# Second phase: z transposed by VectorE and DRAM, the down product three tiles behind

## The chip, the cores and the metric

The kernel runs on one core of a Trainium2 chip. The metric is the device time in microseconds of one execution. Before the change it is 914.69 us, the median of three runs (914.66 to 915.95).

## The reference

Retention (batch 4, 8 heads, 768 positions, head size 64) is followed by two dense blocks over the 3072 tokens, each with 512 features in and out.

```
state = gamma * state + k_t v_t^T ;  y_t = scale * q_t state        # attention
h = x @ w_in (512 x 2048) ; g = h clamped to [-1, 1] and blended with a square ; x = g @ w_out
h = x @ w_in (512 x 1024)
e = exp(h - max(h)) ; solu = h * e / (sum(e) + 1e-9)
z = (solu - mean) / sqrt(var + 1e-6)
out = (z * g_ln) @ w_out (1024 x 512)
```

Only the second dense block (the last four lines) is touched by the change.

## The kernel before

All products are done in f32 split into a high and a low part (`split`, `passes`): a product is three matmuls, hi x hi, hi x lo and lo x hi, so the splits of every operand are made by ScalarE (the high part, a copy that rounds) and by VectorE or POOL (the low part, a subtraction).

The first phase (`first_phase`) does attention and the first dense block for six blocks of 512 tokens and stores its result x2, transposed, in DRAM. In its last block it also loads and splits the weights of the second dense block.

The second phase (`second_phase`) goes over 24 tiles of 128 tokens. For each tile:
- TensorE `up(t, n)`: h for 128 tokens x 1024, in two halves of 512 columns, 12 matmuls each, into one of two PSUM tensors `h2_0`, `h2_1`. It waits for `h2_used` of tile t-2, that is for solu of that tile.
- VectorE and ScalarE in turn: `h_max` (L787), `neg_max` (L789), exp on ScalarE (L752), the sum and its inverse (L792, L795), `solu` (L797), `neg_mean` (L800), square on ScalarE (L755), `var` (L805), the power -0.5 on POOL (L818), and `z` (L808).
- TensorE `flip(t)` (L694): eight transposes of 128x128, that is matmuls of z with an identity, into the PSUM tensor `zT_ps`.
- `split_z(t)`: ScalarE copies the two halves of `zT_ps` as `zT_hi` (L727, through the helper `copy`) and VectorE subtracts for `zT_lo` (L776).
- TensorE `down(t)` (L706): 24 matmuls of zT with w_out into `o_ps`; ScalarE copies the result to `o` and SP stores it (L655).

Each engine works through a queue written out by hand. TensorE does up(t, 0), flip(t-1), up(t, 1), down(t-1). VectorE and ScalarE begin tile t with `split_x`, in ten of the tiles (the split of the next pair of x2 tiles, L770 on VectorE), then with split_z(t-1), and go on to tile t. SP loads x2 for two tiles (L650) when the products of an earlier pair have ended, and stores the outputs. In tile 0 the last two down products of the first phase and its evacuations are put in (`finish`).

There is one `z`, one `zT`, and two slots of `o` and `x2`. The SBUF of the second phase lies over weights of the first (`place`).

Of the kernel before, what the change touches and what calls it, by code (L numbers as in the profile page):

```python
# [5 lines left out]
F32 = mybir.dt.float32  # L6
# [54 lines left out]
def place(nc):  # L61
# [26 lines left out]

    plain("ident", [P, P])
    plain("g_ln", [P, FT2])  # L90
# [42 lines left out]
    plain("o", [P, 2, DM])  # L133
    split("zT", [P, FT2, P])
    assert cursor[0] <= w_at + 9 * 8192
    return mem


def first_phase(nc, block, io, sem, mem, x2_dram, finish):
    w, w_raw, x, y, g, gate = (mem[n] for n in ("w", "w_raw", "x", "y", "g", "g_raw"))  # L140
    tables, state, half_bias, ident = (mem[n] for n in ("tables", "state", "half_bias", "ident"))
    kn_scale = tables[:, 0:H]
# [6 lines left out]
    with ExitStack() as ctx:  # L149
# [419 lines left out]
        def _(pool):  # L569
# [28 lines left out]
            def dense(blk):  # L598
                for f in range(FT1):
# [8 lines left out]
                    if blk == BLOCKS - 1 and 12 <= f < FT1:  # L608
                        for piece in (2 * (f - 12), 2 * (f - 12) + 1):
# [4 lines left out]

            nc.gpsimd.memset(ident[:, :], 0.0).then_inc(sem["ident"], 1)
            pool.wait_ge(sem["ident"], 1)
            nc.gpsimd.affine_select(out=ident[:, :], in_=ident[:, :], compare_op=ALU.not_equal, fill=1.0, base=0,
                                    pattern=[[-1, P]], channel_multiplier=1).then_inc(sem["ident"], 1)
            for f in range(W_READY):
# [7 lines left out]

def second_phase(nc, block, io, sem, mem, x2_dram, finish):
# [3 lines left out]
    w_in, w_out, g_ln = mem["w2_in"], mem["w2_out"], mem["g_ln"]  # L632
    x_raw, x = [mem["x2_0_raw"], mem["x2_1_raw"]], [mem["x2_0"], mem["x2_1"]]
    e, solu, dev, z, zT, o, power, ident = (
        mem[n] for n in ("e", "solu", "dev", "z", "zT", "o", "power", "ident"))
    with ExitStack() as ctx:
        hp = [ctx.enter_context(nc.psum_tensor(f"h2_{i}", [P, FF2], F32)) for i in range(2)]
        tp = ctx.enter_context(nc.psum_tensor("zT_ps", [P, FF2], F32))
        op = [ctx.enter_context(nc.psum_tensor(f"o_ps{i}", [P, DM], F32)) for i in range(2)]
# [4 lines left out]
        @block.sync  # L644
        def _(sp):
            def load_x2(n):
                wait(sp, sem["h2_ready"], 4 * n - 4)
                for m in range(KT):
                    wait(sp, sem["x2_stored"][m], 16 * (n // 2 + 1))
                sp.dma_start(x_raw[n % 2][:, :, :], x2_view[:, :, n * 2 * P:(n + 1) * 2 * P])\  # L650
                    .then_inc(sem["x2_loaded"][n % 2], 16)

            def store(t):
                sp.wait_ge(sem["o_ready"], t + 1)
                sp.dma_start(io["out"][t], o[:, t % 2, :]).then_inc(sem["o_stored"][t % 2], 16)  # L655

            for pair in range(TILES // 2):
                if pair + 2 < TILES // 2:
                    load_x2(pair + 2)
                store(2 * pair)  # L660
                store(2 * pair + 1)
            for par in range(2):
                sp.wait_ge(sem["o_stored"][par], 16 * (TILES // 2))

        @block.tensor
        def _(pe):
            mm = nc.tensor.matmul

            def up(t, n):
                if n == 0:  # L670
                    if t == 0:
                        pe.wait_ge(sem["probs"], 2 * CHUNKS)
                        pe.wait_ge(sem["y_done"], LATER)
                        pe.wait_ge(sem["state_added"], UPDATES)
                        pe.wait_ge(sem["w2_in_lo"], KT)
                    if t == 1:
                        pe.wait_ge(sem["gmax"], BLOCKS * FT1)
                    wait(pe, sem["h2_used"], t - 1)
                    wait(pe, sem["x2_lo"], t // 2 + 1)
                cols = slice((t % 2) * P, (t % 2 + 1) * P)  # L680
                for kt in range(KT):
                    for i, (xx, ww) in enumerate(passes(x[t // 2 % 2], w_in)):
                        last = mm(hp[t % 2][:, SEGS[n]], xx[:, kt, cols], ww[:, kt, SEGS[n]],  # L683
                                  start=kt == 0 and i == 0, stop=kt == KT - 1 and i == 2)
                last.then_inc(sem["h2_ready"], 1)

            def flip(t):
# [3 lines left out]
                pe.wait_ge(sem["z_ready"], t + 1)  # L691
                wait(pe, sem["zT_lo"], 2 * t)
                for f in range(FT2):
                    last = nc.tensor.transpose(tp[:, f * P:(f + 1) * P], z[:, f * P:(f + 1) * P], ident[:, :])  # L694
                    if f % 4 == 3:
                        last.then_inc(sem["zT_ready"], 1)

            def down(t):
# [24 lines left out]

        @block.scalar
        def _(act):
# [19 lines left out]
            for t in range(TILES):  # L745
                if t >= 2 and t % 2 == 0 and t // 2 + 1 < TILES // 2:
                    split_x(t // 2 + 1)
                if t:
                    split_z(t - 1)
                act.wait_ge(sem["neg_max"], t + 1)  # L750
# [6 lines left out]
                if t == 0:  # L757
                    finish["act_evacuate"]()
                else:
                    output(t - 1)  # L760
            split_z(TILES - 1)
            output(TILES - 1)

        @block.vector
        def _(dve):
# [7 lines left out]
            def split_z(t):  # L773
                for n in range(2):
                    dve.wait_ge(sem["zT_hi"], 2 * t + n + 1)
                    tt(zT[1][:, 4 * n:4 * n + 4, :], tp[:, SEGS[n]].rearrange("p (f t) -> p f t", f=4),  # L776
                       zT[0][:, 4 * n:4 * n + 4, :].bitcast(F32), ALU.subtract).then_inc(sem["zT_lo"], 1)

            dve.wait_ge(sem["power_set"], 1)
            for t in range(TILES):  # L780
                if t >= 2 and t % 2 == 0 and t // 2 + 1 < TILES // 2:
                    split_x(t // 2 + 1)
                if t:
                    split_z(t - 1)
                h = hp[t % 2][:, :]
# [16 lines left out]
                if t == 0:  # L802
# [19 lines left out]
SEMAPHORES = {  # L822
    1: ("first_mask mask_loaded tables gains ident half_set power_set state_zeroed x0_hi x0_lo "
        "kn_scaled s_ready probs y_ready y_done ku_ready state_added state_decayed w_hi w_in_lo w_out_lo "
        "x_hi x_lo h_ready clamped squared gmax g_hi g_lo g_used "
        "w2_in_hi w2_in_lo w2_scaled w2_out_hi w2_out_lo x2_hi x2_lo h2_ready h2_used z_ready zT_ready zT_hi "
        "zT_lo o_done o_ready h_max neg_max e_ready e_sum_eps e_inv neg_mean sq_sum var rstd"),
    2: "acc_free x2_loaded o_stored",
    4: "x2_stored w2_in_loaded",
# [6 lines left out]
def build(nc, io):  # L836
    x2_dram = nc.dram_tensor("x2T", (DM, TOKENS), F32).ap()
    with ExitStack() as ctx:
        sem = {}
# [57 lines left out]
```

## Time and profile before

| | us |
|---|---|
| median of three runs | 914.69 |
| profiled execution, its own time | 917.66 |
| its span, first to last instruction | 915.9 |
| TensorE busy (PE) | 898.3 |
| VectorE busy (DVE) | 386.5 |
| ScalarE busy (ACT) | 281.9 |
| POOL busy | 211.9 |

The mean granted clock of TensorE is 0.996 of full speed. The second phase begins at about 617 us. In the profile, PE is TensorE, PEld its weight loads, DVE is VectorE, ACT is ScalarE, POOL is GpSimd and SPq the queue of SyncE, which issues the DMAs. The durations of successive matmuls overlap, so the distance between their starts tells how long one holds the engine.

### The profile page before, as it was taken

The numbers are of one execution on the slowest core, as the hardware profiler recorded it, in microseconds if no ns is written. First come the engines' busy times: TensorE is split into PE (matmuls) and PEld (weight loads), VectorE is DVE, ScalarE is ACT, GpSimd is POOL, SyncE is SP. The second block draws the span as 40 slices with busy tenths as digits, with TensorE's granted clock in tenths as the row PEclk, the third lists the DMA queues.
The fourth block names the chain that finished last, engine by engine and source line by source line (L and its number), as shares of the span: only waits on it lengthen the run. The fifth ranks groups of instructions, "written<-read, shape, count | busy, mean of one in ns | idle before, by whom it ended". The sixth has DMA issues, their size and how long they took to land.

```text
span 915.9 us, 12101 instructions
## 1 busy us (share of the span) xinstructions
PE 898.3 (98%) x5056; PEld 742.2 (81%) x5056; DVE 386.5 (42%) x642; ACT 281.9 (31%) x438; POOL 211.9 (23%) x187
## 2 busy tenths in 40 slices
PE   6999999999999999999999999999999999999997
PEld 5788888888888888888888888887888888888885
DVE  4544443334333343334322343535554455445542
ACT  2433332213212232122212243343333333333332
POOL 2554532322222322322212122252000000000000
PEclk9999999999999999999999999999999999999998
DMA  9812111111121111110111032202111111111100
GB/s 346 320 59 70 47 47 47 48 57 35 58 69 59 47 47 47 56 49 24 58 58 35 1 108 93 76 1 70 47 47 47 43 37 37 47 47 47 47 24 23
DMA packets 33462, 57.68 MB, mean 63 GB/s; under 512 B 3328, under 2 KB 9472, under 8 KB 33408
## 3 DMA queue, kind: packets, MB, share of 16 engines
q1 hardware_dynamic: 33120, 56.38, 17.9%
q8 instruction: 40, 0.66, 0.3%
q10 hardware_dynamic: 288, 0.53, 0.2%
q14 instruction: 14, 0.11, 0.0%
HBM read 44.31 MB, written 12.58 MB: 62 GB/s over the span
## 4 chain that ended last, share of the span: by engine, by line
PE 95%; issue 2%; DVE 1%; ACT 1%; POOL 1%; DMA 1%; POOLq 0%; SPq 0%; ACTq 0%
PE acc L338 30%; PE h L325 28%; PE h L683 14%; PE o_ps L706 13%; PE att L266 3%; PE att L279 2%; PE zT_ps L694 2%; PE att L282 2%; PE att L295 1%; DMA q<-in_q 1%; POOL w L595 0%; PE acc L279 0%; PE h L266 0%; ACT w L365 0%; POOL kn L576 0%
## 5 line engine op out<-in xcount | busy, mean ns | idle before, releaser
L338 PE MATMUL acc<-g_hi,w 128*128 128x512 f32 x768 | 256.7, 395 | 0.0
L325 PE MATMUL h<-x_hi,w 128*128 128x512 f32 x768 | 252.4, 390 | 3.9 <-DVE x_lo L454 2.1
L604 POOL TENSOR_TENSOR g_lo<-g_raw,g_hi 128x512 fp32r<-128x512 f32 x96 | 123.2, 1284 | 404.9 <-ACT g_hi L365 404.9
L414 ACT ACTIVATE g_raw<-g_raw,half_bias 128x512 f32<-128x512 f32 x96 | 69.5, 724 | 348.0 <-DVE g_raw L539 348.0
L325 PEld LDWEIGHTS h<-x_hi,w 128*128 128x128 f32 x768 | 144.2, 188 | 34.4 <-ACT x_hi L365 2.4
L338 PEld LDWEIGHTS acc<-g_hi,w 128*128 128x128 f32 x768 | 144.1, 188 | 33.2 <-issue 0.7
L338 PE MATMUL acc<-g_lo,w 128*128 128x512 f32 x384 | 149.8, 390 | 0.0
L325 PE MATMUL h<-x_lo,w 128*128 128x512 f32 x384 | 149.4, 389 | 0.0
L539 DVE TENSOR_SCALAR g_raw<-h 128x512 f32<-128x512 f32 x96 | 66.4, 691 | 185.1 <-PE acc L338 184.4
L544 DVE TENSOR_TENSOR g_raw<-h,g_raw 128x512 f32<-128x512 f32 x96 | 66.4, 692 | 62.3 <-ACT g_raw L414 61.7
L325 PEld LDWEIGHTS h<-x_lo,w 128*128 128x128 f32 x384 | 72.1, 188 | 14.9
L338 PEld LDWEIGHTS acc<-g_lo,w 128*128 128x128 f32 x384 | 72.1, 188 | 13.9
L365 ACT ACTIVATE g_hi<-g_raw 128x512 fp32r<-128x512 f32 x96 | 60.7, 632 | 72.8 <-DVE g_raw L544 72.8
L706 PE MATMUL o_ps<-w_out_hi,zT_hi 128*128 128x512 f32 x192 | 75.8, 395 | 1.7 <-DVE zT_lo L776 1.7
L683 PE MATMUL h<-w_in_hi,x_hi 128*128 128x512 f32 x192 | 76.6, 399 | 0.0
L706 PE MATMUL o_ps<-w_out_hi,zT_lo 128*128 128x512 f32 x192 | 75.4, 393 | 0.0
L706 PE MATMUL o_ps<-w_out_lo,zT_hi 128*128 128x512 f32 x192 | 75.4, 393 | 0.0
L683 PE MATMUL h<-w_in_hi,x_lo 128*128 128x512 f32 x192 | 75.0, 391 | 0.0
L683 PE MATMUL h<-w_in_lo,x_hi 128*128 128x512 f32 x192 | 74.8, 390 | 0.0
L818 POOL TENSOR_TENSOR rstd<-var,power 128x1 f32<-128x1 f32 x24 | 13.1, 548 | 263.3 <-DVE var L805 263.3
L752 ACT ACTIVATE e<-h,neg_max 128x1024 f32<-128x1024 f32 x24 | 26.8, 1117 | 84.0 <-DVE neg_max L789 84.0
L776 DVE TENSOR_TENSOR zT_lo<-zT_ps,zT_hi 128x512 fp32r<-128x512 f32 x48 | 31.0, 687 | 32.3 <-ACT zT_hi L727 32.2
(72 smaller groups left out, 899.4 us busy)
## 6 DMA issues: line engine op xcount, KB each, us to landing
kT<-in_kT SPq DMA_DIRECT2D x24, 256.0 KB, 2.7
q<-in_q SPq DMA_DIRECT2D x24, 256.0 KB, 2.7
v<-in_v SPq DMA_DIRECT2D x24, 256.0 KB, 2.9
x2T<-y SPq DMA_DIRECT2D x24, 256.0 KB, 2.5
x_raw<-x2T SPq DMA_DIRECT2D x12, 512.0 KB, 3.7
out<-o SPq DMA_DIRECT2D x24, 256.0 KB, 2.0
kn<-in_kn SPq DMA_DIRECT2D x20, 256.0 KB, 3.6
w_raw<-in_moe_w_in SPq DMA_DIRECT2D x16, 256.0 KB, 9.5
```

Of the source, the lines that this page charges most:

```text
L266: last = mm(out[e][:, p * P:(p + 1) * P], kT[half(e), p, :], q[half(e), p, :], start=True, stop=True)
L325: last = mm(hb[f % 2][:, :], ww, xx[:, kt, :], start=kt == 0 and t == 0, stop=kt == KT - 1 and t == 2)
L338: last = mm(acc[m][:, :], ww, gg[:, f % 2, :], start=f == 0 and t == 0, stop=f == FT1 - 1 and t == 2)
L365: return nc.scalar.activation(out, in_, ACT.Copy)
L414: nc.scalar.activation(gate[:, f % 2, :], gate[:, f % 2, :], ACT.Square, bias=half_bias[:, 0:1], scale=0.5).then_inc(sem["squared"], 1)
L539: nc.vector.tensor_scalar(gate[:, f % 2, :], h, 1.0, -1.0, ALU.min, ALU.max)\
L544: tt(gate[:, f % 2, :], h, gate[:, f % 2, :], ALU.max).then_inc(sem["gmax"], 1)
L604: tt(g[1][:, f % 2, :], gate[:, f % 2, :], g[0][:, f % 2, :].bitcast(F32), ALU.subtract)\
L683: last = mm(hp[t % 2][:, SEGS[n]], xx[:, kt, cols], ww[:, kt, SEGS[n]], start=kt == 0 and i == 0, stop=kt == KT - 1 and i == 2)
L706: last = mm(op[t % 2][:, :], zz[:, f, :], ww[:, f, :], start=f == 0 and i == 0, stop=f == FT2 - 1 and i == 2)
L752: nc.scalar.activation(e[:, :], hp[t % 2][:, :], ACT.Exp, bias=st("neg_max", t), accum_out=st("e_sum", t)).then_inc(sem["e_ready"], 1)
L776: tt(zT[1][:, 4 * n:4 * n + 4, :], tp[:, SEGS[n]].rearrange("p (f t) -> p f t", f=4), zT[0][:, 4 * n:4 * n + 4, :].bitcast(F32), ALU.subtr ...
```

## The change

TensorE no longer transposes. VectorE transposes z in squares of 32x32, right behind z, into `zq` (`zq[i*32+r, q, f, c]`, where i is the group of 32 tokens and q the group of 32 features within 128). SP stores `zq` (512 KB) to DRAM, waits until it has landed, and loads it in four DMAs of 128 KB, one for each group of 32 partitions, in runs of 1 KB, as `zt`, in which the 32-token groups stand side by side. ScalarE and VectorE split `zt`, now from SBUF, into one of three `zT`. `zq` and `zt` have two slots.

The down product of tile t-3 (`LAG2`) now follows the whole up product of tile t. VectorE does split_z(t-1) at the end of tile t, behind the transpose of z(t); ScalarE does it at the end of tile t too, behind square(t) and the output of tile t-3. On SP the turn of tile t stands behind the store of output t-3. The identity and its two POOL instructions go. Without `zT_ps`, `o_ps0` and `o_ps1` come to lie two PSUM banks earlier.

```diff
+LAG2 = 3
+SQ = 32
@@ place
-    split("zT", [P, FT2, P])
-    assert cursor[0] <= w_at + 9 * 8192
+    plain("zq", [P, 2, P // SQ, FT2, SQ])
+    plain("zt", [P, 2, P // SQ, FT2, SQ])
+    for n in range(LAG2):
+        split(f"zT{n}", [P, FT2, P])
+    assert cursor[0] <= w_at + 13 * 8192
@@ first_phase, POOL
-            nc.gpsimd.memset(ident[:, :], 0.0).then_inc(sem["ident"], 1)
-            pool.wait_ge(sem["ident"], 1)
-            nc.gpsimd.affine_select(out=ident[:, :], ...)
@@ second_phase, SP
-            for pair in range(TILES // 2):
-                if pair + 2 < TILES // 2:
-                    load_x2(pair + 2)
-                store(2 * pair)
-                store(2 * pair + 1)
+            def turn(t):
+                sp.wait_ge(sem["zq_ready"], t + 1)
+                wait(sp, sem["zt_loaded"][t % 2], 64 * (t // 2))
+                sp.dma_start(z_dram[t % 2], zq[:, t % 2, :, :, :].rearrange("p q f c -> p (q f c)"))\
+                    .then_inc(sem["zq_stored"][t % 2], 16)
+                sp.wait_ge(sem["zq_stored"][t % 2], 16 * (t // 2 + 1))
+                wait(sp, sem["zT_lo"], 2 * t - 2)
+                squares = z_dram[t % 2].rearrange("(i r) (q x) -> q r i x", r=SQ, q=P // SQ)
+                for q in range(P // SQ):
+                    sp.dma_start(zt[q * SQ:(q + 1) * SQ, t % 2, :, :, :].rearrange("r i f c -> r i (f c)"),
+                                 squares[q]).then_inc(sem["zt_loaded"][t % 2], 16)
+
+            for t in range(TILES):
+                if t % 2 and t // 2 + 2 < TILES // 2:
+                    load_x2(t // 2 + 2)
+                if t >= LAG2:
+                    store(t - LAG2)
+                turn(t)
+            for t in range(TILES - LAG2, TILES):
+                store(t)
@@ second_phase, TensorE
-                up(t, 0)
-                if t >= 2:
-                    flip(t - 1)
-                up(t, 1)
+                up(t)
                 if t == 0:
                     finish["down"]()
-                if t == 1:
-                    flip(0)
-                if t:
-                    down(t - 1)
-            flip(TILES - 1)
-            down(TILES - 1)
+                if t >= LAG2:
+                    down(t - LAG2)
+            for t in range(TILES - LAG2, TILES):
+                down(t)
@@ second_phase, ScalarE
             def split_z(t):
-                wait(act, sem["o_done"], t)
+                act.wait_ge(sem["zt_loaded"][t % 2], 64 * (t // 2 + 1))
+                wait(act, sem["o_done"], t - LAG2 + 1)
                 for n in range(2):
-                    act.wait_ge(sem["zT_ready"], 2 * t + n + 1)
-                    copy(zT[0][:, 4 * n:4 * n + 4, :], tp[:, SEGS[n]].rearrange("p (f t) -> p f t", f=4))\
-                        .then_inc(sem["zT_hi"], 1)
+                    fs = slice(4 * n, 4 * n + 4)
+                    copy(zT[t % LAG2][0][:, fs, :].rearrange("p f (i c) -> p f i c", c=SQ),
+                         zt[:, t % 2, :, fs, :].rearrange("p i f c -> p f i c")).then_inc(sem["zT_hi"], 1)
...
-                if t:
-                    split_z(t - 1)
                 act.wait_ge(sem["neg_max"], t + 1)
...
-                else:
-                    output(t - 1)
+                if t >= LAG2:
+                    output(t - LAG2)
+                if t:
+                    split_z(t - 1)
+            output(TILES - 3)
             split_z(TILES - 1)
+            output(TILES - 2)
             output(TILES - 1)
@@ second_phase, VectorE
-                if t:
-                    split_z(t - 1)
                 h = hp[t % 2][:, :]
...
+                dve.wait_ge(sem["z_ready"], t + 1)
+                wait(dve, sem["zq_stored"][t % 2], 16 * (t // 2))
+                nc.vector.transpose(zq[:, t % 2, :, :, :].rearrange("p q f c -> p f q c"),
+                                    z[:, :].rearrange("p (f q c) -> p f q c", q=P // SQ, c=SQ))\
+                    .then_inc(sem["zq_ready"], 1)
+                if t:
+                    split_z(t - 1)
             split_z(TILES - 1)
```

## Rows read from the trace of the kernel before

**Rows 1.** The page: busy time by engine, and the chain's shares.
```profile
PE 898.3 (98%) x5056; PEld 742.2 (81%) x5056; DVE 386.5 (42%) x642; ACT 281.9 (31%) x438; POOL 211.9 (23%) x187
...
PE 95%; issue 2%; DVE 1%; ACT 1%; POOL 1%; DMA 1%; POOLq 0%; SPq 0%; ACTq 0%
```

**Rows 2.** Timeline, a steady tile on TensorE: start us, us, engine, line, operation.
```profile
785.03 1.03 PE L694 MATMUL zT_ps<-ident,z 128*128 128x128 f32 x8
...
788.64 0.39 PE L706 MATMUL o_ps<-w_out_hi,zT_hi 128*128 128x512 f32 x1
...
794.08 0.39 PE L683 MATMUL h<-w_in_hi,x_hi 128*128 128x512 f32 x1
...
796.82 1.04 PE L694 MATMUL zT_ps<-ident,z 128*128 128x128 f32 x8
```

**Rows 3.** Timeline, tiles 0 and 1.
```profile
622.48 0.39 PE L338 MATMUL acc<-g_hi,w 128*128 128x512 f32 x1
...
631.81 0.81 DVE L808 TENSOR_SCALAR z<-solu,neg_mean,rstd 128x1024 f32<-128x1024 f32 x1 [0.74 <-POOL rstd L818]
...
633.13 0.39 PE L683 MATMUL h<-w_in_hi,x_lo 128*128 128x512 f32 x1
...
635.37 0.50 PE L706 MATMUL o_ps<-w_out_hi,zT_hi 128*128 128x512 f32 x1 [0.98 <-DVE zT_lo L776]
```

**Rows 4.** Timeline, the end on TensorE.
```profile
899.88 0.39 PE L706 MATMUL o_ps<-w_out_hi,zT_lo 128*128 128x512 f32 x1
...
905.08 0.77 PE L706 MATMUL o_ps<-w_out_hi,zT_hi 128*128 128x512 f32 x1 [0.71 <-DVE zT_lo L776]
...
909.06 0.48 PE L706 MATMUL o_ps<-w_out_hi,zT_hi 128*128 128x512 f32 x1
...
912.36 0.39 PE L706 MATMUL o_ps<-w_out_hi,zT_lo 128*128 128x512 f32 x1
```

**Rows 5.** Busy time by stretch, the end (PEclk: granted clock).
```profile
901.00:916.00 15.00, 9.64 (x32) 7.46 (x32) 2.19 (x3) 1.96 (x4) 0.50 (x1) 0.77 0.09 35
```

**Rows 6.** Timeline, a steady tile on VectorE.
```profile
786.36 1.29 DVE L776 TENSOR_TENSOR zT_lo<-zT_ps,zT_hi 128x512 fp32r<-128x512 f32 x2 [0.68 <-ACT zT_hi L727]
...
788.84 1.22 DVE L787 TENSOR_REDUCE h_max<-h 128x1 f32<-128x1024 f32 x1 [1.20 <-PE h L683]
...
791.91 1.28 DVE L797 SCALAR_TENSOR_TENSOR solu<-e,e_inv,h 128x1024 f32<-128x1024 f32 x1
...
795.52 0.81 DVE L808 TENSOR_SCALAR z<-solu,neg_mean,rstd 128x1024 f32<-128x1024 f32 x1 [0.66 <-POOL rstd L818]
```

**Rows 7.** Groups by line of VectorE and POOL: busy us, mean ns.
```profile
L770 DVE TENSOR_TENSOR x_lo<-x_raw,x_hi 128x1024 fp32r<-128x1024 f32 x10 | 12.2, 1219 | 0.0
...
L524 DVE TENSOR_TENSOR x_lo<-x_raw,x_hi 128x1024 fp32r<-128x1024 f32 x1 | 1.5, 1472 | 1.6 <-ACT x_hi L365 1.6
...
L604 POOL TENSOR_TENSOR g_lo<-g_raw,g_hi 128x512 fp32r<-128x512 f32 x96 | 123.2, 1284 | 404.9 <-ACT g_hi L365 404.9
```

**Rows 8.** DMAs: median us to landing by line, four issues in row, the x2 load.
```profile
out<-o SPq DMA_DIRECT2D x24, 256.0 KB, 2.0
...
x2T<-y SPq DMA_DIRECT2D x4, 256.0 KB, 3.1
...
631.40 1.88 SPq L202 DMA_DIRECT2D x2T<-y  x4
...
L650 SPq DMA_DIRECT2D x_raw<-x2T x10: 371/377/378, 633.6 to 847.7; - x10
...
DMA to landing us min/median/max: 3.5/3.6/4.9
```

**Rows 9.** ScalarE: the output copy in a tile, groups of copies.
```profile
794.58 0.57 ACT L727 ACTIVATE o<-o_ps 128x512 f32<-128x512 f32 x1
...
L365 ACT ACTIVATE g_hi<-g_raw 128x512 fp32r<-128x512 f32 x96 | 60.7, 632 | 72.8 <-DVE g_raw L544 72.8
...
L727 ACT ACTIVATE zT_hi<-zT_ps 128x512 fp32r<-128x512 f32 x48 | 26.2, 595 | 47.0 <-PE zT_ps L694 47.0
```

More of the change, by code:

```diff
@@ L87, in split_in_place @@
         mem[f"{name}_raw"] = put(f"{name}_raw", shape, F32, at=at)
-    plain("ident", [P, P])
     plain("g_ln", [P, FT2])
@@ L140, in first_phase @@
     w, w_raw, x, y, g, gate = (mem[n] for n in ("w", "w_raw", "x", "y", "g", "g_raw"))
-    tables, state, half_bias, ident = (mem[n] for n in ("tables", "state", "half_bias", "ident"))
+    tables, state, half_bias = (mem[n] for n in ("tables", "state", "half_bias"))
     kn_scale = tables[:, 0:H]
@@ L625, in _, with second_phase @@
                 dense(blk)
-def second_phase(nc, block, io, sem, mem, x2_dram, finish):
+def second_phase(nc, block, io, sem, mem, x2_dram, z_dram, finish):
     TILES = TOKENS // P
@@ L631, in second_phase @@
     x2_view = x2_dram.rearrange("(kt p) t -> p kt t", p=P)
-    w_in, w_out, g_ln = mem["w2_in"], mem["w2_out"], mem["g_ln"]
+    w_in, w_out = mem["w2_in"], mem["w2_out"]
     x_raw, x = [mem["x2_0_raw"], mem["x2_1_raw"]], [mem["x2_0"], mem["x2_1"]]
-    e, solu, dev, z, zT, o, power, ident = (
-        mem[n] for n in ("e", "solu", "dev", "z", "zT", "o", "power", "ident"))
+    e, solu, dev, z, zq, o, power = (mem[n] for n in ("e", "solu", "dev", "z", "zq", "o", "power"))
+    zT, zt = [mem[f"zT{n}"] for n in range(LAG2)], mem["zt"]
     with ExitStack() as ctx:
         hp = [ctx.enter_context(nc.psum_tensor(f"h2_{i}", [P, FF2], F32)) for i in range(2)]
-        tp = ctx.enter_context(nc.psum_tensor("zT_ps", [P, FF2], F32))
         op = [ctx.enter_context(nc.psum_tensor(f"o_ps{i}", [P, DM], F32)) for i in range(2)]
@@ L667, in _, with up, down @@
             mm = nc.tensor.matmul
[L669 to L675, printed above, removed]
-                    if t == 1:
-                        pe.wait_ge(sem["gmax"], BLOCKS * FT1)
-                    wait(pe, sem["h2_used"], t - 1)
-                    wait(pe, sem["x2_lo"], t // 2 + 1)
-                cols = slice((t % 2) * P, (t % 2 + 1) * P)
[L681 to L687, printed above, removed]
+            def up(t):
+                if t == 0:
+                    pe.wait_ge(sem["probs"], 2 * CHUNKS)
+                    pe.wait_ge(sem["y_done"], LATER)
+                    pe.wait_ge(sem["state_added"], UPDATES)
+                    pe.wait_ge(sem["w2_in_lo"], KT)
+                if t == 1:
+                    pe.wait_ge(sem["gmax"], BLOCKS * FT1)
+                wait(pe, sem["h2_used"], t - 1)
+                wait(pe, sem["x2_lo"], t // 2 + 1)
+                cols = slice((t % 2) * P, (t % 2 + 1) * P)
+                for seg in SEGS:
+                    for kt in range(KT):
+                        for i, (xx, ww) in enumerate(passes(x[t // 2 % 2], w_in)):
+                            last = mm(hp[t % 2][:, seg], xx[:, kt, cols], ww[:, kt, seg],
+                                      start=kt == 0 and i == 0, stop=kt == KT - 1 and i == 2)
+                last.then_inc(sem["h2_ready"], 2)
+            def down(t):
                 if t == 0:
@@ L690, in flip @@
                         pe.wait_ge(sem["acc_free"][par], 2 * BLOCKS)
[L691 to L698, printed above, removed]
                 wait(pe, sem["o_ready"], t - 1)
@@ L704, in down @@
                         pe.wait_ge(sem["w2_out_lo"], f + 1)
-                    for i, (zz, ww) in enumerate(passes(zT, w_out)):
+                    for i, (zz, ww) in enumerate(passes(zT[t % LAG2], w_out)):
                         last = mm(op[t % 2][:, :], zz[:, f, :], ww[:, f, :],
@@ L774, in split_z @@
                 for n in range(2):
+                    fs = slice(4 * n, 4 * n + 4)
                     dve.wait_ge(sem["zT_hi"], 2 * t + n + 1)
-                    tt(zT[1][:, 4 * n:4 * n + 4, :], tp[:, SEGS[n]].rearrange("p (f t) -> p f t", f=4),
-                       zT[0][:, 4 * n:4 * n + 4, :].bitcast(F32), ALU.subtract).then_inc(sem["zT_lo"], 1)
+                    hi, lo = (part[:, fs, :].rearrange("p f (i c) -> p f i c", c=SQ) for part in zT[t % LAG2])
+                    tt(lo, zt[:, t % 2, :, fs, :].rearrange("p i f c -> p f i c"), hi.bitcast(F32), ALU.subtract)\
+                        .then_inc(sem["zT_lo"], 1)
             dve.wait_ge(sem["power_set"], 1)
@@ L822 @@
 SEMAPHORES = {
[L823 removed]
+    1: ("first_mask mask_loaded tables gains half_set power_set state_zeroed x0_hi x0_lo "
         "kn_scaled s_ready probs y_ready y_done ku_ready state_added state_decayed w_hi w_in_lo w_out_lo "
         "x_hi x_lo h_ready clamped squared gmax g_hi g_lo g_used "
[L826 removed]
+        "w2_in_hi w2_in_lo w2_scaled w2_out_hi w2_out_lo x2_hi x2_lo h2_ready h2_used z_ready zq_ready zT_hi "
         "zT_lo o_done o_ready h_max neg_max e_ready e_sum_eps e_inv neg_mean sq_sum var rstd"),
[L828 removed]
+    2: "acc_free x2_loaded o_stored zq_stored zt_loaded",
     4: "x2_stored w2_in_loaded",
@@ L837, in build @@
     x2_dram = nc.dram_tensor("x2T", (DM, TOKENS), F32).ap()
+    z_dram = [nc.dram_tensor(f"z{n}", (P, FF2), F32).ap() for n in range(2)]
     with ExitStack() as ctx:
@@ L847, in build @@
         first_phase(nc, block, io, sem, mem, x2_dram, finish)
-        second_phase(nc, block, io, sem, mem, x2_dram, finish)
+        second_phase(nc, block, io, sem, mem, x2_dram, z_dram, finish)
 def kernel(q, k, v, moe_w_in, moe_w_out, moe2_w_in, moe2_w_out, moe2_g_ln):
```

3 lines of the change are left out of this document (removed).

## The prediction

> **What bounds the kernel now.** I read the page's busy shares and chain first, then the second phase closely, since nothing before 617 us changes but two small POOL instructions. TensorE is busy 98% of the span and is 95% of the chain that ended last [rows 1]: its instructions set the time, and other engines matter only where it waits. In a steady tile TensorE never stops: 24 products take 794.08 - 788.64 = 5.44 us (0.2267 each), so a tile's 48 cost 10.88; a tile is 796.82 - 785.03 = 11.79 long; the other 0.91 is the eight transposes [rows 2]. So they are paid in full on the bounding engine, though they overlap among themselves (eight in 1.03).
>
> **The sum for TensorE.** What is not product in the second phase:
> - Start: up(1) ends at 633.13 + 0.23 = 633.36, the first down product starts at 635.37: 2.0 us of flip(0) and of the wait for zT_lo [rows 3].
> - Steady: from 635.37 + 5.44 = 640.81 to 899.88 + 0.23 = 900.11 lie 22 flips and 22 x 10.88 = 239.4 us of products; the other 19.9 is 0.90 a tile [rows 3, 4].
> - End: from 900.11 to 905.08 TensorE waits for z(23), flips and waits for zT_lo: 5.0 us. The last 24 products then take 912.59 - 905.08 = 7.51 instead of 5.44: their first nine start 0.43 apart (the granted clock of this stretch is 0.77, so part of it ran at 1.2 GHz), 2.1 us [rows 4, 5].
>
> Together 29.0 us. Check: from 622.48 (up(0) done) 48 half tiles of 5.44 are 261.1, ending at 883.6; plus 29.0 is 912.6, where the trace has it. With TensorE never waiting the span would be 883.6 + 3.3 (912.59 to the end of the span: output copy and store [rows 4]) = 886.9, or 29.0 less: the most that the change can give.
>
> **What the change puts in place of it: VectorE.** One new VectorE pass (T) a tile, a round trip through DRAM (R), and the split copies now read SBUF. T isn't in the trace. VectorE passes over 128x1024 f32 take 1.22 (the reduce of h_max), 1.22 (x_lo) and, the scaling that makes z, 0.81; 1.47 is the slowest; far off, POOL needs 1.28 for 512, that is 2.57 for 1024 [rows 6, 7]. So the bounds are 0.8 and 2.6; I take T = 1.25, a little above the two at 1.22, which it is nearest to: one tensor read and one written, in blocks.
>
> VectorE's queue in a tile, counted from D(t), the start of h_max(t):
> - z ends at D + 7.49 (788.84 to 795.52 + 0.81) [rows 6]; the passes between wait for ScalarE's exp and square and for POOL's power, and don't change.
> - + 0.04 + T transpose, - 0.08 (an independent successor starts that much early: two halves of 0.69 show as 1.29 [rows 6]) + 1.29 split_z(t-1), - 0.08: D(t+1) = D(t) + 8.66 + T = 9.91.
> - before ten of the tiles also split_x, 1.22 - 0.08 = 1.14 [rows 7]: 11.05.
>
> The mean is 10.43, against 10.88 of TensorE: VectorE is 96% filled and nearly the bound, where it had over 1 us a tile free. It also starts late: the new order gives TensorE up(1), up(2), up(3) back to back (633.36, 638.80, 644.24), while z(0) ends at 632.62 [rows 3], h_max(1) starts at 633.8, h_max(2) at 633.8 + 9.91 + 1.14 = 644.9, 6 us behind its product, h_max(3) at 654.8, 10.6 behind. Does TensorE feel it? up(4) starts at 644.24 + 5.44 = 649.7 and needs solu(2), done 4.4 us after h_max starts (791.91 + 1.28 against 788.84 [rows 6]), at 649.3: just in time. Then the lag shrinks, since VectorE is faster than TensorE. down(t-3), due when up(t) ends, needs split_z(t-3), which is done before h_max(t-1): enough. So I take no stall from tile 1 to 22.
>
> **The round trip R**, from the transpose's end to the last of four loads landed, behind one another on SP. The store is 512 KB: stores of 256 KB land 2.0 to 3.1 us after issue, the 512 KB load 3.6 (4.9 at most); I take 3.3. The four loads are issued about 0.45 apart (four x2T stores take 1.88) and the last (128 KB) lands 2.0 to 3.1 after its issue; I take 1.35 + 2.3. With 0.15 of SP between: R = 7.1; the ends are 2.0 + 1.35 + 2.0 + 0.1 = 5.5 and 4.9 + 1.4 + 4.9 + 0.1 = 11.3 [rows 8].
> R is hidden in the middle. ScalarE comes to split_z(t-1) at D(t) + 6.3, after square and output (794.58 + 0.57 in a tile with D = 788.84) [rows 9], that is 9.91 + 6.3 - 8.78 = 7.4 us after the transpose of t-1 ended; VectorE wants the first half at D(t) + 8.7, so ScalarE may start 1.8 later still. So R up to 9.2 costs nothing before the last tile. On SP the x2 load goes out behind the four loads, and the store of an output and the turn of the next tile behind it: it may land up to 1 us after ScalarE wants it, in ten tiles; with VectorE's lag that would cost up to 0.5 each, and I count 0.5 in all. The copies out of SBUF cost 0.63 instead of 0.60 [rows 9], beside other waits: nothing. POOL's two identity instructions at the start go: at most POOL's 1% of the chain, nearly all of it in later work, so nothing [rows 1]. Nobody else waits for the swap of PSUM banks.
>
> **The end.** D(23) = 633.8 + 22 x 9.91 + 10 x 1.14 = 863.3, + 0.5 = 863.8; up(23) ends at 644.24 + 20 x 10.88 = 861.8. z(23) at 871.3, transposed 872.6, landed 879.7, first half copied and split 881.1 (0.60 + 0.69 + 0.1). TensorE has down(20), (21), (22) until 861.8 + 3 x 5.44 = 878.2, so it waits 2.9 us before down(23), which ends at 886.5; + 3.3 = 889.8. That is 26.1 below the span of 915.9. After the wait of 2.1 us and the transposes the clock had fallen in the run before; a wait of 2.9 may do the same, 0 to 2.1 us, and I take 1. So -25.1. The profiled execution took 917.66 us (its span and 1.76 around it), 2.97 above the median of the runs shown; I carry the difference to the median: 914.69 - 25.1 = 889.6.
>
> **The rivals.**
> 1. *The transpose pass is dear* (T well over 1.3). VectorE's queue is the pace, so each us of T above 1.25 costs 22 steps and the last tile, 23 to 24 us in all, one for one. T = 1.8 gives 889.6 + 13 = 903; T = 2.5 gives 918, slower than before; the break is at T = 2.3. For it: no row shows the operation, and the POOL row shows that a pass can need twice the time for an element. Against it: every VectorE pass over 1024 elements lies at or below 1.47 [rows 7]. The Trainium skill ("VectorE: DVE Perf Modes", The three transpose paths) gives 311 ns for 128 columns in bf16; times eight, an estimate by that page, is 2.49 us, and the kernel would be no faster. The Trainium skill elsewhere ("Vector Engine (DVE) Microarchitecture Reference", 3.8 The reshape front-end and per-opcode configuration) has the transpose at one element per cycle and lane, by which most of the 311 ns are fixed and T is an estimated 1.2 to 1.3; the trace of before decides neither.
> 2. *The round trip sets the pace* (R over 9.2), the one that can turn the sign by itself. ScalarE's queue then stops at split_z(t-1), and VectorE's behind it: D(t+1) = D(t-1) + 8.78 + R + 0.1 + 1.8, and 1.14 more in every other tile, so (R + 11.8)/2 a tile. R = 10 gives 10.9, 22 x 0.5 + 2.9 at the end + 2 at the start = 16 us, 905; R = 11 gives 11.4 and 25 + 3: 918, slower; it decides from R = 10.9. For it: the 4.9 us seen for a 512 KB load, and x2 loads and output stores on the same queue. Against it: 3.6 is the median of that load, and 2.0 that of the stores [rows 8]. The Trainium skill ("VectorE: DVE Perf Modes", The three transpose paths) warns that a plain DMA that transposes by strides is 19 times slower than the crossbar; here the rows moved are 1 KB whole, as in the x2 load that lands in 3.6 us [rows 8], so I don't apply it; if it held, it would be this rival.
> 3. *TensorE keeps most of its tile*: the pitch of 0.2267 is not kept where the transposes went, or VectorE's lag costs stalls in every tile (11.3 instead of 10.88): 22 x 0.4 = 9 us given back, 899. Against it: the 24 products beside VectorE and ScalarE work keep the pitch exactly [rows 2].
>
> **How the numbers follow.** The forecast 0.66; rival 1 0.14 (half of it under 903, 0.04 past the break); rival 2 0.13 (0.06 past the break); rival 3 0.07. The least is 914.69 - 29 = 885.7 (no wait at the end); the forecast's own range is 886 to 895 (T to 1.4, R to 8.5, clock 0 to 2). To hold 8 in 10 it reaches into rivals 1 and 3: 886 to 903. A difference under 0.2% (1.8 us) can't be told from none here. Faster by more: 0.66 + 0.07 + 0.09 + 0.06 = 0.88; within: 0.02; slower: 0.10.
>
> **What would show it.** Right: no L694 and a TensorE tile of 10.88 from tile 4 on; the VectorE transpose at 1.2 to 1.3 us; h_max 6 to 11 us behind its product at tiles 2 to 6 and under 3 at tile 23; four loads landed 6.5 to 8.5 us after the transpose; one wait of 2 to 4 us before the last down product and 9 or fewer slow products behind it. Wrong: waits of TensorE for solu or zT_lo in every tile (rival 1 if VectorE has no idle time before h_max, rival 2 if ScalarE waits for the loads), or a pitch over 0.23.

## The result, and the profile after

The changed kernel takes 890.2 us (median of four runs, 890.07 to 890.45) against 915.32 for the kernel before on the same chip: a ratio of 0.9713, with a 95% interval of 0.970 to 0.9727. The forecast was 889.6. Executions of the changed kernel differ by about 1.2 us with the mean granted clock, 1.00 or 0.998, so a difference under 1 us between two kernels here is none. The profiled execution has a span of 888.7 us, 27.2 under the 915.9 of the trace before.

The page of the changed kernel, busy time and chain, which answer to [rows 1]:

```profile
PE 873.4 (98%) x4864; PEld 719.5 (81%) x4864; DVE 411.9 (46%) x666; ACT 283.0 (32%) x438; POOL 211.6 (24%) x185
...
PE 67%; DVE 18%; issue 5%; ACT 4%; DMA 3%; POOL 2%; SPq 1%; POOLq 0%; ACTq 0%; DVEq 0%
```

TensorE is as full as before and has 192 instructions less. But the chain is now on VectorE, ScalarE and POOL for 24% of the span, most of the second phase: it is the chain through VectorE's queue, which just keeps up.

The timeline of TensorE: the start of up(2), the turns between down and up at the start, the start of down(20), and the rows with a wait:

```profile
632.72 0.39 PE L700 MATMUL h<-w_in_hi,x_hi 128*128 128x512 f32 x1
...
643.60 0.39 PE L715 MATMUL o_ps<-w_out_hi,zT_hi 128*128 128x512 f32 x1
...
649.52 0.50 PE L700 MATMUL h<-w_in_hi,x_hi 128*128 128x512 f32 x1 [0.32 <-DVE solu L804]
...
655.12 0.39 PE L715 MATMUL o_ps<-w_out_hi,zT_hi 128*128 128x512 f32 x1
660.56 0.39 PE L700 MATMUL h<-w_in_hi,x_hi 128*128 128x512 f32 x1
666.00 0.39 PE L715 MATMUL o_ps<-w_out_hi,zT_hi 128*128 128x512 f32 x1
...
861.84 0.39 PE L715 MATMUL o_ps<-w_out_hi,zT_hi 128*128 128x512 f32 x1
...
879.78 0.47 PE L715 MATMUL o_ps<-w_out_hi,zT_hi 128*128 128x512 f32 x1 [1.47 <-DVE zT_lo L785]
...
885.12 0.39 PE L715 MATMUL o_ps<-w_out_hi,zT_lo 128*128 128x512 f32 x1
```

A tile is 666.00 - 655.12 = 10.88 us, where it was 11.79 [rows 2]; from 655.12 to 861.84 there are 19 of them in 206.72 us, 10.88 each, and no wait. What is left that is not product: up(4) should start at 643.60 + 5.44 = 649.04 and down(1) follow at 654.48; it follows at 655.12, so 0.64 there. down(20) starts at 861.84, so the last of the 24 down products should start at 861.84 + 3 x 5.44 = 878.16 and starts at 879.78: 1.62. It takes 5.57 instead of 5.44. Together 2.4 us, where the kernel before had 29.0. That is 26.6 of the 27.2; the other 0.6 is the first phase, which ends at 616.4 instead of 617.0 (TensorE's first wait for a DMA and its waits for a weight were shorter), and isn't the change's: a second trace of the kernel before has 616.6.

VectorE, three tiles at the start and the last:

```profile
632.01 1.25 DVE L819 STREAM_TRANSPOSE zq<-z 128x1024 f32<-128x1024 f32 x1
...
645.11 1.22 DVE L794 TENSOR_REDUCE h_max<-h 128x1 f32<-128x1024 f32 x1
...
654.97 1.22 DVE L794 TENSOR_REDUCE h_max<-h 128x1 f32<-128x1024 f32 x1
...
862.37 1.22 DVE L794 TENSOR_REDUCE h_max<-h 128x1 f32<-128x1024 f32 x1
...
869.89 1.25 DVE L819 STREAM_TRANSPOSE zq<-z 128x1024 f32<-128x1024 f32 x1
871.06 1.25 DVE L785 TENSOR_TENSOR zT_lo<-zt,zT_hi 128x512 fp32r<-128x512 f32 x2
878.94 1.29 DVE L785 TENSOR_TENSOR zT_lo<-zt,zT_hi 128x512 fp32r<-128x512 f32 x2 [6.63 <-ACT zT_hi L731]
```

h_max(2) starts 6.9 us after its product ended (638.16), h_max(3) 11.4 after (643.60), h_max(23) 0.5 after (861.84). The lag builds up in the first three tiles and is worked off by the last. Before the change h_max waited 26.3 us in all for its products; now it never waits for one: but for 0.9 us at split_x(2), VectorE goes from tile to tile at its own pace, in 9.86 us, or 11.00 where split_x comes first.

SP and ScalarE around the last round trip:

```profile
871.17 0.34 SPq L662 DMA_DIRECT2D z<-zq  x1
873.80 1.75 SPq L668 DMA_DIRECT2D zt<-z  x4
```

```profile
878.28 1.15 ACT L731 ACTIVATE zT_hi<-zt 128x512 fp32r<-128x512 f32 x2 [4.77 <-DMA zt<-z]
```

The transpose ends at 871.14, ScalarE goes on at 878.28: R = 7.1.

### The profile page after: what moved, and what is told of

Its sections match the earlier page's. It is cut to its first block, busy times and chain, and to the rows that moved or that the text cites. A ratio compares the mean times of both kernels' runs of the same rounds, so it can differ in the third digit from the quotient of the medians.

```text
span 888.7 us, 11899 instructions
## 1 busy us (share of the span) xinstructions
PE 873.4 (98%) x4864; PEld 719.5 (81%) x4864; DVE 411.9 (46%) x666; ACT 283.0 (32%) x438; POOL 211.6 (24%) x185
## 2 busy tenths in 40 slices
DMA packets 50742, 82.84 MB, mean 93 GB/s; under 512 B 5248, under 2 KB 23680, under 8 KB 50688
## 4 chain that ended last, share of the span: by engine, by line
PE 67%; DVE 18%; issue 5%; ACT 4%; DMA 3%; POOL 2%; SPq 1%; POOLq 0%; ACTq 0%; DVEq 0%
PE acc L342 30%; PE h L329 29%; DVE solu L804 3%; DVE zq L819 3%; ACT e L755 3%; DVE h_max L794 3%; DVE zT_lo L785 3%; PE att L270 2%; PE att L283 2%; DVE z L815 2%; PE att L286 2%; POOL rstd L832 1%; DVE x_lo L777 1%; DMA mask<-in_mask 1%; PE att L299 1%
## 5 line engine op out<-in xcount | busy, mean ns | idle before, releaser
L700 PE MATMUL h<-w_in_hi,x_hi 128*128 128x512 f32 x192 | 74.8, 390 | 0.3 <-DVE solu L804 0.3
L715 PEld LDWEIGHTS o_ps<-w_out_hi,zT_hi 128*128 128x128 f32 x192 | 36.0, 188 | 9.4 <-issue 1.9
```

What stands on the lines that cost most here:

```text
L700: last = mm(hp[t % 2][:, seg], xx[:, kt, cols], ww[:, kt, seg], start=kt == 0 and i == 0, stop=kt == KT - 1 and i == 2)
L715: last = mm(op[t % 2][:, :], zz[:, f, :], ww[:, f, :], start=f == 0 and i == 0, stop=f == FT2 - 1 and i == 2)
```

## The experiments

Twelve runs were made, on three chips. "The changed kernel" below is e_after_again, its repeat on the chip of e_no_dram, e_pe_transpose_lag and e_last_two_queues. On the two chips of the others the kernel before takes 916.2 us, 0.3 more than the 915.9 there; each ratio is against the kernel before on the same chip. Three dots stand for lines that aren't shown.

**The reference again.** No edit.

> The changed kernel itself, unaltered, on the chip of the next three kernels, as their reference: 890.2 us, 24 to 25 us under the kernel before. If the 27.2 us between the two profiled spans were the usual difference it would be 888.

Measured: 891.1 us (889.9 to 891.2), ratio 0.9725 (0.9712 to 0.9739), against 915.9 before. The usual difference is 24.8, not the 27.2 of the two profiles.

**The kernel before, profiled again.** No edit.

> The kernel before, once more with a profile, for its end: in the trace read for the prediction the clock had fallen for the last down product (7.5 us instead of 5.4), and that execution lay 3 us above the median. If the median execution keeps the clock there, this span is 913 to 914 and the last product takes 5.4 to 6.5; if not, the 3 us lie elsewhere.

Measured: 916.4 us, span 914.6. Its end on TensorE:

```profile
902.00 1.09 PE L694 MATMUL zT_ps<-ident,z 128*128 128x128 f32 x8 [2.14 <-DVE z L808]
904.22 0.76 PE L706 MATMUL o_ps<-w_out_hi,zT_hi 128*128 128x512 f32 x1 [1.13 <-DVE zT_lo L776]
904.78 0.63 PE L706 MATMUL o_ps<-w_out_lo,zT_hi 128*128 128x512 f32 x1
...
908.15 0.39 PE L706 MATMUL o_ps<-w_out_lo,zT_hi 128*128 128x512 f32 x1
...
911.11 0.39 PE L706 MATMUL o_ps<-w_out_hi,zT_lo 128*128 128x512 f32 x1
```

The eight transposes take 1.09 here and 1.97 in the first trace, the last product 911.34 - 904.22 = 7.1 here and 7.5 there, and the first phase is 0.4 shorter: 0.5 + 0.4 + 0.4 is the 1.3 us between the two spans. So the clock falls at the end in this execution too, later and for less, and the first trace lies 1 to 3 us above other executions. Spans of 912.9 with a mean clock of 1.00 occur; there it can hardly have fallen, but they have no trace.

**Without DRAM.** ScalarE and VectorE split zq itself, no DMA; the squares stand in the wrong places, so the output isn't the reference's.

```diff
-                turn(t)
...
-                act.wait_ge(sem["zt_loaded"][t % 2], 64 * (t // 2 + 1))
+                act.wait_ge(sem["zq_ready"], t + 1)
...
-                wait(dve, sem["zq_stored"][t % 2], 16 * (t // 2))
...
-    zT, zt = [mem[f"zT{n}"] for n in range(LAG2)], mem["zt"]
+    zT, zt = [mem[f"zT{n}"] for n in range(LAG2)], mem["zq"]
```

> The changed kernel without the way through DRAM: ScalarE and VectorE split zq itself, as soon as it is transposed (the squares stand in the wrong places, so the output is not the reference's). Theory (the round trip of 7.1 us is hidden in the middle and shows only before the last down product): 1.5 to 1.9 us less than the changed kernel, 888.5. Rival (the DMA traffic or ScalarE's waits for it cost something in every tile): 3 us less or more, 887 or below, and passes of VectorE or ScalarE that are shorter than before.

Measured: 889.4 us (888.3 to 889.9), 1.7 under the changed kernel; profiled spans 886.1 and 888.1. TensorE has no wait at all in the second phase. The groups on VectorE, first without DRAM, then the changed kernel's:

```profile
L784 DVE TENSOR_TENSOR zT_lo<-zq,zT_hi 128x512 fp32r<-128x512 f32 x48 | 30.1, 665 | 2.1 <-ACT zT_hi L730 2.1
```

```profile
L785 DVE TENSOR_TENSOR zT_lo<-zt,zT_hi 128x512 fp32r<-128x512 f32 x48 | 30.1, 667 | 6.6 <-ACT zT_hi L731 6.6
L819 DVE STREAM_TRANSPOSE zq<-z 128x1024 f32<-128x1024 f32 x24 | 29.9, 1246 | 0.8
```

The extra 25 MB of traffic (82.84 MB on the page of the changed kernel, 57.68 on the page of before) cost the passes nothing, and the whole way through DRAM costs about 2 us, at tile 4 and before the last product. The theory holds.

**T doubled.** The same transpose once more, into a spare buffer, ahead of the real one.

```diff
+    plain("spare", [P, P // SQ, FT2, SQ])
...
+                nc.vector.transpose(mem["spare"][:, :, :, :].rearrange("p q f c -> p f q c"),
+                                    z[:, :].rearrange("p (f q c) -> p f q c", q=P // SQ, c=SQ))
                 nc.vector.transpose(zq[:, t % 2, :, :, :].rearrange("p q f c -> p f q c"),
```

> The changed kernel with a second VectorE transpose of the same size in each tile, into a spare buffer, ahead of the real one: T doubled. Theory (rival 1 of the prediction: VectorE's queue is the pace from the first tile to the last): 1.17 us in each of 22 steps and at the end, 27 us more, 917. Rival (TensorE's tile of 10.88 has room for it, VectorE being busy 60% only): under 900.

Measured: 917.25 us (916.4 to 918.4), ratio 1.001 (0.9999 to 1.002): 26.1 more than the changed kernel, from 24 added passes of 1.246 us, 29.9 us in all. VectorE's last tiles:

```profile
866.21 1.22 DVE L795 TENSOR_REDUCE h_max<-h 128x1 f32<-128x1024 f32 x1
877.18 1.22 DVE L795 TENSOR_REDUCE h_max<-h 128x1 f32<-128x1024 f32 x1
888.16 1.22 DVE L795 TENSOR_REDUCE h_max<-h 128x1 f32<-128x1024 f32 x1
```

10.98 a tile, where the changed kernel has 9.86 without split_x: 1.12 more, and 23 such steps are 25.8 us. In the steady tiles of the changed kernel VectorE is busy for 66 to 68% of the time, and yet it takes the added pass at nearly full price: 3.2 us of a tile are its waits for ScalarE's exp and square and for POOL's power, which the added pass doesn't fill. This is rival 1 made true. Its price of 23 to 24 us for each us holds when the us is one of the tile's length (26.1 by 1.12 is 23).

**The order alone.** The kernel before, with three zT and down three tiles behind; TensorE still transposes, flip(t-1) inside up(t).

```diff
+    for n in range(LAG2):
+        split(f"zT{n}", [P, FT2, P])
...
-                if t:
-                    down(t - 1)
-            flip(TILES - 1)
-            down(TILES - 1)
+                if t >= LAG2:
+                    down(t - LAG2)
+            down(TILES - 3)
+            flip(TILES - 1)
+            down(TILES - 2)
+            down(TILES - 1)
```

> The kernel before with the order of the changed one alone: down three tiles behind, three zT, TensorE still transposes (flip(t-1) inside up(t), flip(23) behind down(21)). Theory (each flip costs 0.90 us of TensorE wherever it stands, the lag hides only the waits at both ends): start 1.1 and end 4.1 us saved, 2.1 more where the clock had fallen at the end: 908.5 to 910. So taking the transposes off TensorE alone is worth about 19. Rival (the flip is expensive for its waits and the order alone frees most of it): under 900.

Measured: 927.25 us (924.9 to 927.7), ratio 1.0117 (1.0101 to 1.0133): slower than before by 11, where I had expected 6 to 7 faster. Both theories fail. TensorE's waits:

```profile
643.72 1.97 PE L698 MATMUL zT_ps<-ident,z 128*128 128x128 f32 x8 [6.22 <-DVE z L816]
...
656.42 1.77 PE L698 MATMUL zT_ps<-ident,z 128*128 128x128 f32 x8 [4.86 <-DVE z L816]
```

With three up products back to back VectorE falls behind as in the changed kernel, but flip(t-1) asks for z when half of up(t) is done, 2.7 us after its start. TensorE waits 11.1 us in all, and its matmuls behind the waits are slow (1.97 for eight transposes, against 1.03). Waits and slow matmuls make 13.8 us, and the 6.8 us of waits and slow products at the two ends of the kernel before are gone; that gives 7.0 of the 7.2 us between this span and the first of the kernel before (923.1 against 915.9). The traced execution is the fastest of its four; what the others lose beyond it, at granted clocks of 0.989 to 0.993, has no trace.

**The order alone, z asked for late.** The same with flip(t-2) inside up(t) and three z.

```diff
-                if t >= 2:
-                    flip(t - 1)
+                if t >= 2:
+                    flip(t - 2)
...
```

> The order of the changed kernel with TensorE's transposes, as e_pe_transpose_lag, which was 11 us slower than the kernel before and whose TensorE waited 6.2 and 4.9 us for z at tiles 2 and 3. Here flip(t-2) stands inside up(t) instead of flip(t-1), with three z. Theory (the order needs that TensorE asks for z late, since VectorE lags 6 to 11 us behind at the start; then only the flips themselves are left, 24 x 0.90): no wait for z, 908.5 + 1.8 = 910 us, 5 to 6 under the kernel before and 19 to 20 above the changed one. Rival (something else in the three-tile order costs): 915 or more.

Measured: 911.85 us (910.7 to 912.3), ratio 0.9953 (0.9936 to 0.9971), one wait of TensorE of 0.9 us. So the order is worth 4.3 us (0.5%) by itself, once TensorE asks for z late, and taking the 24 flips off TensorE the other 20.7 (24 x 0.90 = 21.6, less what the round trip leaves at the end).

**Two tiles behind.**

```diff
-LAG2 = 3
+LAG2 = 2
-            output(TILES - 3)
```

> The changed kernel with the down product two tiles behind instead of three. Theory (the third tile covers VectorE's late start and the last round trip): TensorE waits 4.3 us before down(0) and 1.1 before down(1), and 6 to 6.6 instead of 1.5 before the last down product, after which the clock may have fallen: 10 to 12.5 us more than the changed kernel, 901 to 903. Rival (two tiles are enough, since the round trip is 7.1 us and a tile 10.9): within 2 us of the changed kernel.

Measured: 902.6 us (901.1 to 903.8), ratio 0.9848 (0.9826 to 0.9871), 11.5 more than the changed kernel. TensorE's waits:

```profile
644.05 0.77 PE L715 MATMUL o_ps<-w_out_hi,zT_hi 128*128 128x512 f32 x1 [4.43 <-DVE zT_lo L784]
...
885.23 0.47 PE L715 MATMUL o_ps<-w_out_hi,zT_hi 128*128 128x512 f32 x1 [4.09 <-DVE zT_lo L784]
...
893.17 0.47 PE L715 MATMUL o_ps<-w_out_hi,zT_hi 128*128 128x512 f32 x1 [0.60 <-DVE zT_lo L784]
```

The first wait is the one expected, 4.4 us before down(0). The others aren't: none stands before down(1), and instead of 6 us before the last product there are 4.1 before down(22) and 0.6 before down(23). The clock takes the rest: up(3) starts 8.45 us after down(0) (granted clock 0.61 from 644 to 652 us), and down(23) 7.9 after down(22), 0.6 of it the wait, where 5.44 is usual. So the total was right, and its parts only in the main. The third tile is worth these 11.5 us.

**R lengthened.** zq is stored twice before the loads.

```diff
+                for again in range(2):
+                    sp.dma_start(z_dram[t % 2], zq[:, t % 2, :, :, :].rearrange("p q f c -> p (q f c)"))\
+                        .then_inc(sem["zq_stored"][t % 2], 16)
+                    sp.wait_ge(sem["zq_stored"][t % 2], 16 * (2 * (t // 2) + again + 1))
...
```

> The changed kernel with zq stored twice, one after the other, before the loads: R goes from 7.1 to 9.8, past the 9.2 of the prediction. Theory (past it a tile takes (R + 11.8)/2 = 10.8 on VectorE instead of 10.43): 22 x 0.35 = 7.6 and 2.7 at the end, 10 us more, 901; ScalarE waits for zt in most tiles. Rival (still hidden, since 10.8 is under TensorE's 10.88): only the 2.7 us at the end, 893.5.

Measured: 924.4 us (923.6 to 925.7), ratio 1.0093 (1.0074 to 1.0112): 33 more than the changed kernel, three times what I expected. SP in two tiles:

```profile
703.29 2.95 SPq L663 DMA_DIRECT2D z<-zq  x2
708.54 1.74 SPq L669 DMA_DIRECT2D zt<-z  x4
710.46 0.38 SPq L652 DMA_DIRECT2D x_raw<-x2T  x1
710.88 0.50 SPq L657 DMA_DIRECT2D out<-o  x1
713.14 4.74 SPq L663 DMA_DIRECT2D z<-zq  x2
720.17 1.75 SPq L669 DMA_DIRECT2D zt<-z  x4
```

A line with x2 at its end lasts from the first issue to the end of the second, so 2.95 means that the first store landed after 2.6 us, 4.74 that it took 4.4; this one went out 2.7 us behind an x2 load. The two tiles have a different R: from zq's end at 703.27 to 712.95, where ScalarE goes on, it is 9.7, as expected; from 713.12 to 724.81 it is 11.7. What VectorE waits for in these two tiles is on these lines, ScalarE first:

```profile
712.95 1.15 ACT L732 ACTIVATE zT_hi<-zt 128x512 fp32r<-128x512 f32 x2 [2.29 <-DMA zt<-z]
715.67 1.06 ACT L732 ACTIVATE x_hi<-x_raw 128x1024 fp32r<-128x1024 f32 x1 [1.57 <-DMA x_raw<-x2T]
...
724.81 1.16 ACT L732 ACTIVATE zT_hi<-zt 128x512 fp32r<-128x512 f32 x2 [0.60 <-DMA zt<-z]
```

```profile
713.62 1.29 DVE L786 TENSOR_TENSOR zT_lo<-zt,zT_hi 128x512 fp32r<-128x512 f32 x2 [0.50 <-ACT zT_hi L732]
716.77 1.23 DVE L778 TENSOR_TENSOR x_lo<-x_raw,x_hi 128x1024 fp32r<-128x1024 f32 x1 [1.86 <-ACT x_hi L732]
```

The tile with R = 11.7 holds up nobody: VectorE, late by then, doesn't wait for it. The two tiles take 726.67 - 703.27 = 23.4 us. The prediction's form for two tiles, R + 10.68 + 1.14, gives 21.5 with the R of 9.7 that counts; the other 1.9 are the wait for x_hi, which the form doesn't have. Over the whole phase VectorE waits 13.9 us for zT_hi before the last tile's (22.7 in all, 8.8 of it at the end) and 13.3 for x_hi, where the changed kernel has 0 and 0.9. So the round trip was about as long as expected where it counted, and the x2 load, pushed back on SP, cost as much again.

**The same, x2 loads on POOL's queue.**

```diff
-                if t % 2 and t // 2 + 2 < TILES // 2:
-                    load_x2(t // 2 + 2)
@@ POOL, before the power of tile t
+                if t % 2 and t // 2 + 2 < TILES // 2:
+                    load_x2(t // 2 + 2)
...
```

> As e_two_stores, which cost 33 us where I expected 10, but the x2 loads of the second phase are issued from POOL's queue as soon as their slot is free, instead of on SP behind the loads of zt. Theory (the first thing late was not zt but the x2 load, which SP issues behind the turn of the tile before and whose landing then falls into the next store): 901 to 906, tiles of equal length again. Rival (the second store itself makes the round trip much longer than 9.8): 915 or more, with ScalarE waiting for zt as long as before.

Measured: 921.9 us (920.1 to 927.5), ratio 1.0067 (1.0043 to 1.009). My theory fails in its number: ScalarE no longer waits for x2, VectorE waits 1.8 us for x_hi instead of 13.3, and the kernel is hardly faster. The time has moved to the other wait: VectorE waits 23.7 us for zT_hi before the last tile's, instead of 13.9.

```profile
749.95 5.76 SPq L656 DMA_DIRECT2D z<-zq  x2
758.05 1.74 SPq L662 DMA_DIRECT2D zt<-z  x4
```

```profile
747.82 1.12 POOL L824 DMA_DIRECT2D x_raw<-x2T  x1
```

```profile
762.51 1.15 ACT L723 ACTIVATE zT_hi<-zt 128x512 fp32r<-128x512 f32 x2 [5.20 <-DMA zt<-z]
```

The x2 load now goes out 2.1 us ahead of the store in the tile that VectorE waits for, and the first store takes 5.4 us here, the longest, and 3.4 to 3.7 in the eight other such tiles, instead of 2.6. R is 12.6 here (749.92 to 762.51) and 10.5 to 11.6 there. With it the form holds: it gives 24.4 us for these two tiles, which take 24.6 (zq ends at 749.92 and at 774.55). Where the x2 load meets the store, the store is longer, with the load on either queue. It isn't the x2 load alone: stores that go out 0.5 to 1.5 us behind the last load of zt take 3.2 to 3.8 too. That two stores without any x2 load near would cost the expected 10 us wasn't tried.

**Is there more to get?** The last tile's four loads on two queues (SP and ScalarE's), and two variants with the store in halves, each half's loads sent as soon as it has landed.

```diff
...
@@ e_last_two_queues, ScalarE, before the last split_z
+            for q in range(2, P // SQ):
+                act.dma_start(zt[q * SQ:(q + 1) * SQ, last, :, :, :].rearrange("r i f c -> r i (f c)"),
+                              squares[q]).then_inc(sem["zt_loaded"][last], 16)
@@ e_halves, SP
+                for g in range(2):
+                    sp.dma_start(z_dram[t % 2][:, g * 512:(g + 1) * 512],
+                                 zq[:, t % 2, 2 * g:2 * g + 2, :, :].rearrange("p q f c -> p (q f c)"))\
+                        .then_inc(sem["zq_stored"][2 * (t % 2) + g], 16)
...
```

> Only the last tile: two of the four loads of zt are issued from ScalarE's queue beside the two on SP. Theory (the last wait of TensorE is the round trip's end, and the four issues stand 0.43 apart): 0.8 us less than the changed kernel, 889.4, with a last wait of 0.7 instead of 1.5. Rival (the last load's landing is bound by bytes, not by its issue): no difference.

> A candidate for a faster kernel: the changed one with the store of zq in two halves, each of whose loads go out as soon as it has landed, and the x2 loads on POOL's queue. Theory (what is left above TensorE's products is 0.3 us at tile 4 and 1.3 to 1.5 before the last down product, which is R's end; R falls from 7.1 to 6.3): 0.8 to 1.2 us less than the changed kernel, 889.3 to 889.8 where it ran 890.2 to 891.1, last wait 0.3 to 0.7. Rival (the 512 KB take their time whatever the order): no difference.

> The same store in two halves, with the x2 loads left on SP. Theory: the same 0.8 us, since the x2 load only delays VectorE while it lags anyway. Rival (the x2 load's waits, 3 to 4 us of ScalarE's time in all, reach the end): 0.4 us more than e_halves_pool_x.

Measured, in this order: 890.6 us (889.8 to 893.7); 890.5 (889.9 to 892.3); 890.1 (889.6 to 890.4). Ratios 0.9728, 0.9717 and 0.9709, all with intervals that hold the changed kernel's. The last waits are 1.2, 1.0 and 0.9 us, where the changed kernel has 1.3 to 1.5. With two queues the loads go out from 873.59 on and ScalarE goes on at 877.83, 4.2 us later; from SP alone it was 4.4 to 4.5. So the loads' landing is hardly bound by their issue, as its rival said. The two halves shorten the last R from 7.1 to 6.6 and 6.9, not to 6.3. Whether the x2 queue matters can't be told at this size. Nothing beats the changed kernel measurably; what is left above TensorE's products is 1.8 to 2.4 us in its two traces.

## Why the prediction was right

- **What the transposes cost** (0.90 a tile, 29.0 with the waits at both ends): right. 26.6 of the 29.0 are gone in the trace.
- **T = 1.25**: measured 1.246 in all 24 tiles. The nearest rows were those of the full-width passes at 1.22. The estimate of 2.49 by the Trainium skill ("VectorE: DVE Perf Modes", The three transpose paths) doesn't hold when a single instruction takes 1024 columns; one element per cycle and lane (the Trainium skill, "Vector Engine (DVE) Microarchitecture Reference", 3.8) agrees with the 1.246: it lies in the 1.2 to 1.3 that the prediction estimated by that page.
- **VectorE's queue is nearly the bound**: right. 9.86 a tile without split_x (predicted 9.91) and 11.00 with it (11.05). The lag came out at 6.9 and 11.4 (6.1 and 10.6 predicted), since VectorE waited 0.9 us at split_x(2), behind ScalarE's waits for zt(0) and x2; so "just in time" for solu(2) became the 0.64 us at tile 4. Without DRAM that wait is gone, and the 0.64 with it. At tile 23 the lag was 0.5, not 2.0. The doubled pass shows the price: a tile longer by 1.12 us costs 26.1, as rival 1 had it.
- **R = 7.1 at the end**: right; its parts weren't: the store lands in 2.6 (3.3 taken), the last load 3.2 after its issue (2.3 taken). The two errors, of 0.7 and 0.9, nearly cancel: the sum was right by luck.
- **"R up to 9.2 costs nothing"**: shown up to 8.6. At the tiles of the changed kernel where ScalarE waits for zt before the last, R is 7.6 to 7.8, and in e_halves_pool_x it is 8.6 once (654.95 to 663.59); VectorE doesn't wait for zT_hi there. Beyond 9.2 the form (R + 11.8)/2 holds for the R of the tile that VectorE waits for, and lacks the x2 load: with R = 9.7 that load, which SP issues behind the loads of zt, cost as much again. The prediction counted 0.5 us in all for it. In the changed kernel that was enough (ScalarE waited for x2 nine times, 4.4 us in all, VectorE only once); it isn't once the round trip is longer. And R can't be lengthened by a store alone, since the store itself takes longer next to another DMA.
- **The end**: a wait of 1.6 instead of 2.9 (and outside the 2 to 4 given as a sign of being right), and no fall of the clock, for which 1 us was taken. Both errors have the same sign, the 0.64 at tile 4 the other one, and the first phase was 0.6 shorter: the span was forecast 2.1 us too long (890.8 against 888.7).
- **Carrying to the median**: wrong by about as much the other way. The 25.1 were read in the trace of an execution about 2 us above the usual: the usual span of the kernel before is about 914. So 25.1 us forecast and 25.1 measured agree closer than the steps do, by luck: the saving read from the trace was 1.5 us too small for the second phase, and the trace that it started from 2 us too long.
- **What the prediction didn't take apart**: the change has two parts. The order without the move of the transposes costs 11 us, because TensorE then asks for z early in a stretch in which VectorE lags; with z asked for a tile later it gains 4. The round trip through DRAM needs the order: with two tiles of lag instead of three, 11.5 of the 24.8 us are lost.

## What to carry to other kernels

A small operation on the bounding engine is worth its pitch there, here 0.90 us a tile for eight transposes, and can be moved to an engine and a path that take nine times as long, if the consumer is put far enough behind: 1.25 us of VectorE and 7.1 us of DRAM cost 2 us in 890. Before doing it, add up the receiving engine's queue with its waits, not its busy time: VectorE was busy for two thirds of a steady tile and had 0.4 us of it left. And when a product is put several tiles behind, look at the first tiles: the run of products that it lets loose sends the other engines into a lag, which is harmless only if nothing that TensorE does early needs their results.

## What the runs showed of the hardware

- A VectorE transpose in squares of 32x32 over 128x1024 f32 takes 1.246 us, close to the 1.22 of h_max and x_lo and above the 0.81 of the scaling that makes z.
- Four loads of 128 KB take 4.4 to 4.5 us from the first issue when one queue issues them, and 4.2 when two do (one trace).
- A store of 512 KB lands in 2.6 us with no other DMA near. It took 3.3 to 5.4 when it went out 2.1 to 2.7 us behind a 512 KB load (17 stores in e_two_stores and e_two_stores_pool_x, most of them under 4.2), and 5.1 and 6.1 when it went out 1 us behind one.
- After waits of 1.3 and 1.5 us TensorE's products kept their distance of 0.227 in the changed kernel, and after one of 2.07 us in e_two_stores. After 2.1 us, eight transposes and a wait of 0.7 or 1.1, as in both traces of the kernel before, the next 9 and 7 products stood 0.43 apart, which is the lower level of 1.2 GHz; after waits of 4.4 and 4.1 us with two tiles of lag the next 14 and 9 did.
